# Three loads sent together, and VectorE's weight split placed behind a step's sum, maximum and subtraction

## The reference, cut to what matters

```
scores = scale * q_c @ [mem_k, k_ctx].T          # chunks of 32 queries, 16 left, 8 right, 8 memory keys
a = exp(scores - max(scores)); a = a / (sum(a) + 1e-9)
x = a @ [mem_v, v_ctx]                           # attention, 8 heads of 64
h = x @ w_in; y = (h * sigmoid(1.702 * h)) @ w_out   # dense, 512 -> 2048 -> 512
logits = y @ w_gate; e = argmax(logits)          # 8 experts, capacity 384
out[token] = softmax(logits)[e] * (relu(y[token] @ w1[e]) @ w2[e])   # 512 -> 1024 -> 512
```

## Time and profile before

| what | us |
|---|---|
| median of three runs | 506.85 (506.0 to 508.22) |
| profiled execution | 507.59 |
| its span | 505.9 |
| TensorE matmul busy | 488.6 (97%) |
| VectorE busy | 313.1 (62%) |
| ScalarE busy | 219.3 (43%) |
| GpSimd busy | 161.9 (32%) |
| start of the first dense matmul | 23.09 |

### The profile page before, as it was taken

How to read it: one execution, slowest core, us unless ns; L and a number is a source line. 1 busy time by engine, 2 the same in 40 slices (tenths; PEclk the granted TensorE clock), 3 DMA queues, 4 the chain that set the end, 5 groups by cost and what they waited for, 6 DMA issues and landing times.

```text
span 505.9 us, 9477 instructions
## 1 busy us (share of the span) xinstructions
PE 488.6 (97%) x3529; PEld 403.0 (80%) x3529; DVE 313.1 (62%) x677; ACT 219.3 (43%) x384; POOL 161.9 (32%) x190
## 2 busy tenths in 40 slices
PE   8799999999999999999999999999999999999992
PEld 5687888888888887888888778998888878988782
DVE  5476565454257775325777777845578877738960
ACT  3654545443231122113212556324367868846620
POOL 3411010000000000300000037064257999999742
PEclk9999999999999999999999999999999999999997
DMA  7899731498500000201233336125797969947000
GB/s 259 268 269 284 233 108 44 135 326 249 166 1 1 0 2 0 85 0 43 84 90 118 93 135 190 43 90 148 247 351 255 329 259 337 354 152 270 4 28 33
DMA packets 26719, 76.93 MB, mean 152 GB/s; under 512 B 5279, under 2 KB 5279, under 8 KB 26400
## 3 DMA queue, kind: packets, MB, share of 16 engines
q1 hardware_dynamic: 22656, 69.77, 42.2%
q0 software_dynamic: 4000, 6.32, 3.4%
HBM read 62.92 MB, written 19.96 MB: 164 GB/s over the span
## 4 chain that ended last, share of the span: by engine, by line
PE 80%; DMA 6%; DVE 5%; issue 4%; ACT 2%; DVEq 1%; POOL 0%; another core or an unknown queue 0%; SPq 0%; ACTq 0%; POOLq 0%
PE bank L1362 9%; PE bank L1363 9%; PE bank L1364 9%; PE bank L1406 9%; PE bank L1408 9%; PE bank L1407 9%; PE bank L1375 7%; DMA raw<-dense_units 4%; PE bank L1646 3%; PE bank L1377 3%; DMA tile_in<-attention_tiles 3%; PE bank L1648 2%; PE bank L1649 2%; PE bank L1650 2%; PE bank L1353 1%
## 5 line engine op out<-in xcount | busy, mean ns | idle before, releaser
L391 POOL TENSOR_TENSOR w_lo<-raw,w_hi 128x256 fp32r<-128x256 f32 x104 | 90.6, 905 | 13.0 <-ACT w_hi L375 13.0
L665 ACT ACTIVATE g<-bank 128x512 f32<-128x512 f32 x48 | 28.6, 596 | 132.5 <-PE bank L1364 132.5
L391 DVE TENSOR_TENSOR w_lo<-raw,w_hi 128x1024 fp32r<-128x1024 f32 (+1 forms) x60 | 73.4, 1232 | 20.5 <-ACT w_hi L375 19.6
L375 ACT ACTIVATE w_hi<-raw 128x1024 fp32r<-128x1024 f32 x80 | 82.0, 1050 | 5.1 <-DMA raw<-dense_units 5.0
L578 POOL DMA_INDIRECT dispatched_rows<-rows,slot_idx x12 | 12.8, 1071 | 218.5 <-DVE slot_idx L1075 215.8
L1406 PE MATMUL bank<-w_hi,g_hi 128*128 128x512 f32 x192 | 77.2, 402 | 0.0
L1362 PE MATMUL bank<-x_hi,w_hi 128*128 128x512 f32 x192 | 77.1, 402 | 0.0
L1408 PE MATMUL bank<-w_hi,g_lo 128*128 128x512 f32 x192 | 75.8, 395 | 0.0
L1407 PE MATMUL bank<-w_lo,g_hi 128*128 128x512 f32 x192 | 75.8, 395 | 0.0
L1363 PE MATMUL bank<-x_lo,w_hi 128*128 128x512 f32 x192 | 75.7, 394 | 0.0
L1364 PE MATMUL bank<-x_hi,w_lo 128*128 128x512 f32 x192 | 75.6, 394 | 0.0
(11 more groups left out here) (154 smaller groups left out, 815.7 us busy)
## 6 DMA issues: line engine op xcount, KB each, us to landing
raw<-expert_units SPq DMA_DIRECT2D x64, 512.0 KB, 6.6
raw<-dense_units SPq DMA_DIRECT2D x16, 512.0 KB, 5.0
tile_in<-attention_tiles SPq DMA_DIRECT2D x12, 592.0 KB, 5.1
dispatched_rows<-empty SPq DMA_DIRECT2D x26, 257.0 KB, 7.5
slot_rows<-dispatched_rows SPq DMA_DIRECT2D x26, 257.0 KB
tile_in<-attention_tiles SPq DMA_DIRECT2D x12, 384.0 KB, 5.7
gate_rows<-gate_rows SPq DMA_DIRECT2D x2, 1024.0 KB, 5.2
out<-rows,e_token POOLq DMA_INDIRECT x16, 4.2
```

The lines of the kernel that those rows point to most:

```text
L375: act.activation(w_hi[u % RING][:, :], raw[u % RING][:, :], ACT.Copy).then_inc(s_whi, 1)
L391: last = engine.tensor_tensor(w_lo[u % RING][:, part], raw[u % RING][:, part], w_hi[u % RING][:, part].bitcast(F32), ALU.subtract)
```

## The change

Two orders are changed; no instruction is added or removed. On SP, the load of the queries and keys of tile 4 is issued right behind unit 0 and values 2, no longer behind the landing of unit 0. Unit 1 goes out on the landing of unit 0, no longer on that of values 2; the queries and keys of tile 5 go out on the landing of values 2, no longer on that of values 3, which SP no longer waits for. On VectorE, a step's `split_lo` stands behind its `inverse`, `maximum` and `less_max`, ahead of `x_low`.

```diff
             landed_values(0)
             load_unit(0)
             load_values(2)
+            load_queries_keys(FIRST)
             landed_values(1)
             load_values(3)
             landed_unit(0)
-            load_queries_keys(FIRST)
+            load_unit(1)
             landed_values(2)
-            load_unit(1)
-            landed_values(3)
             load_queries_keys(FIRST + 1)
             landed_queries_keys(FIRST)
             unit = 2
...
                 g_low(i)
-                for u in splits_in_step.get(i, []):
-                    split_lo(dve, u)
                 if FIRST <= t < NT - 1:
                     inverse(t + 1)
                 if FIRST + 1 < t + 2 < NT:
                     maximum(t + 2, 0)
                     less_max(t + 2, 0)
+                for u in splits_in_step.get(i, []):
+                    split_lo(dve, u)
                 if FIRST <= t < NT:
                     x_low(t)
```

## The result

The changed kernel takes 510.09 us (median of 8, 508.79 to 513.24) against 506.87 us of the kernel before (median of 8, 505.97 to 508.22). The ratio is 1.0067, 95% interval 1.0042 to 1.0092. I had forecast 506.6 us, in a range of 505.0 to 508.5. The profiled execution took 511.04 us, its span is 509.3.

What follows compares the result with a forecast made beforehand. TensorE, busy 97%, was taken to bound the kernel. A start +0.6 us later, less the 0.86 us gap, plus 0 for the later split, gave -0.26 us on the 506.85 median: 506.6 us, range 505.0 to 508.5.

Steps and rivals of the forecast that it cites:

- What bounds the kernel: Whole span: TensorE, busy 97%, 488.6 of 505.9 us; edits elsewhere help only where it stands still.
- the shift is carried to the end: From the first dense matmul at 23.09 us, TensorE works down a fixed list; the end follows the start one for one.
- The move on VectorE: Steps with split_lo: putting it behind the maximum removes step 2's TensorE wait, -0.86 us, and costs nothing.
- The gap of 0.86 us: TensorE's idle time before step 2's transposes, waiting on less_max(6); forecast to go, -0.86 us.
- the loads' shift would close part of the gap by itself: Step 2: loads up to unit 3 landing likely 1 us sooner would close part of the 0.86 us without VectorE's move.
- Which load pays: SP's queue, served nearly in issue order: unit 0 and values 2 keep their landings, values 3 pay the whole price.
- values 3 pay about 1.6 us: SP's queue: values 3 land near 21.15, not 19.56, so the dense start is 0.6 us later; chance 0.55.
- my upper bound of 2.5 us: Most that values 3 would pay for tile 4's load: 606 KB at 245 GB/s.
- The estimate of 1.4 us: Time added by tile 4's load in SP's queue, by bytes over 436 GB/s behind a fixed part.
- The half clock: TensorE ahead of the dense phase: a granted clock under 1.00 from longer idling would show the forecast wrong; no cost summed.
- My slower rival: Loads in SP's queue share, unit 0 lands later, sum +1.2 us, 508.0; chance 0.20 together with its second form.
- its second form: Values 3 alone pay 2.5 us: start +1.5, less 0.86, sum +0.7 us; within the shared chance 0.20.

Runs made afterwards that it cites:

- experiment 2: The kernel before with only VectorE's new order, loads as before; 506.27 us, ratio 0.9998.
- experiment 1: The changed kernel's three moved loads only, with VectorE's order of the kernel before; 509.86 us, ratio 1.0067 against the kernel before.
- experiments 3: The changed kernel with values 3 issued ahead of tile 4's queries and keys; 507.18 us, ratio 1.0016 against the kernel before.
- experiment 7: The changed kernel with values 3, then tile 4's load, right behind values 2, without waiting for values 1 between; 507.26 us, ratio 1.0010 against the kernel before.
- experiment 6: The changed kernel with only tile 4's load early, unit 1 and tile 5's load waiting as before; 509.97 us, ratio 1.0061 against the kernel before.
- experiment 4: The changed kernel with ten unused matmuls on TensorE ahead of values(3); 507.96 us, ratio 1.0030 against the kernel before.
- experiments 9 to 11: Unused matmuls in TensorE's waits, added to: experiment 7's kernel, 506.19 us; changed kernel with tile 4's load after unit 0's landing, 506.22; kernel before with VectorE's order, 505.59.
- experiment 8: The changed kernel with only tile 4's queries (256 KB) early, its keys on unit 0's landing; 508.26 us, ratio 1.0028 against the kernel before.

## Why the prediction was wrong

*What bounds the kernel, and that the shift is carried to the end: right.* TensorE was 4.69 us late at step 2 and 4.69 us late at 233 us.

*The move on VectorE: right in mechanism.* The gap of 0.86 us goes (experiment 2, in the trace), and the split behind the maximum costs nothing: `x_low(5)` starts at 47.83 with step 2's transposes at 39.29, before at 47.51 with 39.61, so it is 0.64 us later in its step, where I had 0.6, and no new wait of TensorE follows. I also had it that the loads' shift would close part of the gap by itself; experiment 1 shows all of it closed, by TensorE being later and not by the loads being sooner.

*Which load pays: right.* I had values 3 pay and unit 0 not. Unit 0's landing moved by no more than its issue, experiments 3 and 7 free values 3 by the order alone, and experiment 6 pins the loss on tile 4's load. Order of issue in one ring, the rule of the Trainium skill ("DMA: Bandwidth & Descriptors", section "Queues, rings and completion order"), agrees with the order of the landings in experiment 7 at 17.8, 20.7 and 22 us.

*The price of the load: mis-sized.* The step that failed is "values 3 pay about 1.6 us": they landed 4.2 us later (23.72 in place of 19.56), and 3.5 to 3.8 us later where else the load was tried whole (23.32, 23.19, and 23.09 in experiment 4), beyond my upper bound of 2.5 us. The start of `values(3)` moved by 3.6 in place of 1.07 us. I took the price from the first three loads, which nothing else disturbed, and misread them: the matmuls at 4.58 waited for no load. The landings that do show are those of the next two:

```profile
5.94 1.10 PE L1318 MATMUL bank<-tile_in 64*32 64x64 f32 x64 [0.26 <-DMA tile_in<-attention_tiles]
```

and 7.76, so 1.82 us for one load and not 1.59; that is still far from 4.2. I took the bound from the mean rate of the earlier trace rows. By experiment 6 a landing seems to go by the slowest DMA engine, an estimated 2.9 us behind the others there. Why some engine is slower isn't settled. The estimate of 1.4 us by the Trainium skill ("DMA: Bandwidth & Descriptors", section "Anatomy of one DMA — SWDGE (gpsimd) path") is further off still; that section fits single DMAs issued from GpSimd, these are loads of SP with others in flight, and the measurement decides.

*The half clock: left out of the sum.* I named it only as a sign that would prove me wrong, and put it at nothing. It cost 1.9 us on the ratios (experiment 4) and 2.4 us in the traces, as the sum below has it. I had TensorE wait 1.3 us; with 3.09 us and the waits before it the clock fell.

*The sum again,* with measured terms, up to step 2 of the profiled executions. `values(3)` is 3.64 us late; of this 0.46 was free, since tile 4's load held the start before: +3.2 on the start. The clock then takes 27.49 - (23.72 + 2.50 + 0.05) = 1.2 us ahead of the first dense matmul. `hidden(1)` begins at 32.63 in the changed kernel, 5.1 us behind the first dense matmul; in the kernel before, this stretch is 27.06 - 23.09 = 4.0, so +1.2. The gap takes 0.9 off: 3.2 + 1.2 + 1.2 - 0.9 = 4.7 us, which is what was seen at step 2. My slower rival had the right sign and, as its second form, the right place (values 3 alone pay), at +0.7 us.

## What to carry to other kernels

A load that is wanted later, put into the queue ahead of one that is wanted sooner, is paid for by the sooner one. Here it was 6 to 8 us for each MB, where the mean rate of 245 GB/s would say 4; take a price from a mean rate or from undisturbed transfers as a lower bound. Where the delayed load stands in front of TensorE's first long run of work, add the half clock behind the wait as a term of its own, and look at single executions for it: it comes as a longer tail before it moves the median. Where the loads can't be had sooner, a few unused matmuls in such waits can take that tail away: in experiments 9 to 11 none of 36 executions had a mean clock under 0.993, in experiment 7 6 of 11 had. Whether that makes the median faster is shown only where the half clock was in most executions (experiment 4).

## What the runs showed of the hardware that I had not expected

The granted clock fell behind several short waits as well as behind one long: with 1.26, 1.02 and 0.79 us in experiment 8, while the waits of 0.78, 0.26 and 0.83 us in the kernel before left it at 1.00 in the profiled execution. It stayed at half for some 6.8 us in the changed kernel, though TensorE was at work from 23.72 on, and for some 3.4 us in experiment 8.

Four loads in flight from 14 us on, where the kernel before had three, brought none of them in clearly sooner: tile 4's load landed at 22 in both (experiment 7), though the kernel before has the DMA engines at a share of 0.54 from 17.0 to 19.5.
